# Attention, routed experts and gated layers on one core: routing rewritten, expert blocks of 224 tokens

## The chip, the core and the metric

The kernel runs on one core of a Trainium2 chip. A core has five engines with instruction streams of their own: TensorE (PE in the rows; its weight loads are PEld), VectorE (DVE), ScalarE (ACT), GpSimd (POOL) and SyncE (SP, which here only issues DMAs). They meet through semaphores. The metric is the device time of one execution in microseconds, lower is better. Before the change it was 645.58 us, the median of 3 runs (645.01 to 647.66).

## The reference, cut to what matters

```python
# 1. linear attention with decay: r, k, v are [4, 8, 768, 48]; gives x [3072, 384]
# 2. one expert of eight for each token, and only where x @ w_skip > 0
skip_score = x @ w_skip
do_compute = skip_score > 0
xc = x[do_compute]
logits = xc @ w_gate                      # [n, 8]
e_idx = np.argmax(logits, axis=1)
probs = softmax(logits); gate_w = probs[arange, e_idx]
for e in range(8):
    mask = e_idx == e
    h = np.maximum(xc[mask] @ w1[e], 0.0)         # 384 -> 1024
    y[mask] = gate_w[mask, None] * (h @ w2[e])    # 1024 -> 384
out[do_compute] = xc + y
# 3. gated layers on all 3072 tokens
h = (x @ m_w1) * (x @ m_w2) @ w3          # 384 -> 1024 -> 1024
return h @ w_out                          # 1024 -> 384
```

On its own inputs the reference sends 1490 of the 3072 tokens to an expert; the eight experts get 190, 182, 205, 159, 189, 184, 188 and 193 of them.

## The kernel before, in words

Four stages follow each other, each a block of its own; at a block's end all engines wait for each other.

**Attention** works through tiles of 128 rows in a software pipeline (`schedule`). Each finished tile is stored to `xbuf` in DRAM by SP, and TensorE makes nine logits a token from it (eight experts and the skip score). The last part of `lg` is put together when the last tile's logits are there.

**The fold** is independent of the tokens: w3 @ w_out is formed once as `wf`, in 8 chunks of 128 rows. `Fold.turn` transposes chunk i on TensorE (8 transposes), `turned` copies it out on ScalarE, `product` multiplies it by w_out (8 matmuls in four quarters), `taken` copies the result out. Product i waits until product i-1 has been taken. Chunk 0 is turned and multiplied at the end of attention, chunks 1 to 5 are multiplied in routing (1 to 7 turned), chunk 6 after the experts, chunk 7 in the gated layers. The fold's work stands between the steps of routing on TensorE in an order written out by hand.

**Routing** gives each routed token a slot: expert e owns slots from 256e on, and tokens over 256 of an expert go to overflow blocks. VectorE finds the best expert of each token (`mine`, one 0/1 number for each expert and 128 tokens), TensorE counts (ranks within a column, totals), VectorE turns the counts into a slot number `dest` in a chain of small steps, each waiting for the one ahead (`chain`), and splits it into a high part (`hi`, which group of 128 slots) and a low part (`lo`). From them come one-hot tables `oh_hi` and `oh_lo`; `vals` is `oh_hi` times each of five numbers of a token (two make up its number, three its gate), two on VectorE and three on GpSimd (`slot_values`). 24 matmuls `oh_lo` x `vals` then give the lists `slot_token` and `slot_gate`. GpSimd gathers the first expert's tokens by `slot_token` (indirect DMA, two of 128 rows), TensorE transposes them (L1132) and the experts begin.

**Experts**: for each of 8 experts `hidden` (L1146) runs 72 matmuls of 256 columns in four groups of 18, `outputs` (L1159) 2 x 24 matmuls of 384 columns, with the next expert's 6 transposes between the two halves. All are float32r with the operands split in a high and a low part. ScalarE makes the high parts, VectorE the low parts (`hidden_lo`: w2_lo and h_lo for each group; then `w1_lo_`, `x_lo`, `new`), and GpSimd gathers and scatters (`exchange`) and splits one block of the next stage's weights an expert (`wm_lo_`, in experts 0 to 5).

**Gated layers** then run over all tokens in 6 blocks of 512.

## Time and profile before

| | us |
|---|---|
| median of 3 runs | 645.58 |
| the profiled execution's own time | 649.34 |
| its span, first to last instruction | 647.6 |
| attention, up to the block's end | 0 to 138.5 |
| routing, up to the first expert's transposes | 138.8 to 178.5 |
| experts, up to the end of the last outputs | 178.5 to 322.6 |
| the fold's product 6, scatters, gated layers | 322.6 to 647.6 |
| TensorE busy | 613.1 (95%) |

The profiled execution is 3.76 us longer than the median of the runs, and 1.76 us of it lie outside the span. TensorE's granted clock was 1.00 (2.4 GHz) nearly everywhere and 0.50 (1.2 GHz) from 119.5 to 133.1 us. A plain f32 matmul shows as two rows in the timeline (the 8 matmuls of a product are x16), a transpose or a float32r matmul as one.

### The profile page before, as it was taken

The page shows a single profiled execution, that of the slowest core. Times are in us where ns is not written, and L with a number is a line of the kernel's source. Part 1 is how long each engine was busy: PE and PEld are TensorE (multiplying, and loading weights), DVE is VectorE, ACT ScalarE, POOL GpSimd, SP SyncE. Part 2 cuts the span into 40 slices and gives each one's busy share as a digit, 9 for nine tenths or more (in the row PEclk, how much of TensorE's full clock was granted, in tenths as well). Part 3 has the DMA queues.
Part 4 walks back from the last instruction along what each step waited for, and adds up shares of the span by engine and source line. Part 5 has one row for each costly group of instructions (what it writes and reads, how often), then busy time and mean ns, then how long its engine had stood idle before and what let it go on. Part 6 is the DMA issues. An engine that isn't in the chain of part 4 may idle for free. (4 is left out here: it accounts for less than half of the span.)

```text
span 647.6 us, 17433 instructions
## 1 busy us (share of the span) xinstructions
PE 613.1 (95%) x7362; PEld 548.0 (85%) x7362; DVE 302.6 (47%) x464; ACT 217.2 (34%) x382; POOL 155.6 (24%) x182
## 2 busy tenths in 40 slices
PE   7698998689999999999989999999999999999997
PEld 6688888645699999999958898888889888888886
DVE  5477878239377777778412232223214123223222
ACT  2144444212455555555232132122213123213212
POOL 6566777125514444333122000000000000000000
PEclk9899999689999999999999999999999999999999
DMA  9679999546156677764040003002002001001001
GB/s 133 115 145 188 190 187 211 157 128 254 51 172 221 249 266 259 251 222 164 19 153 1 0 1 99 0 1 98 1 1 97 1 1 49 1 0 50 1 0 50
DMA packets 104058, 67.77 MB, mean 105 GB/s; under 512 B 79459, under 2 KB 98053, under 8 KB 104017
## 3 DMA queue, kind: packets, MB, share of 16 engines
q1 hardware_dynamic: 75824, 57.88, 30.8%
q10 hardware_dynamic: 26144, 4.74, 4.3%
q0 software_dynamic: 2048, 4.58, 1.9%
q8 instruction: 29, 0.48, 0.3%
q14 instruction: 13, 0.10, 0.1%
HBM read 56.31 MB, written 12.58 MB: 106 GB/s over the span
## 5 line engine op out<-in xcount | busy, mean ns | idle before, releaser
L1443 DVE TENSOR_TENSOR gl_g_sb<-gl_a_sb,gl_pab 128x512 f32<-128x512 f32 x48 | 33.0, 688 | 187.0 <-ACT gl_a_sb L1420 187.0
L1363 PE MATMUL gl_pab<-gl_xT_hi,wm_lo 128*128 128x512 f32 x288 | 112.9, 392 | 0.0
L1363 PE MATMUL gl_pab<-gl_xT_lo,wm_hi 128*128 128x512 f32 x288 | 112.8, 392 | 0.0
L1363 PE MATMUL gl_pab<-gl_xT_hi,wm_hi 128*128 128x512 f32 x288 | 112.3, 390 | 0.0
L1420 ACT ACTIVATE gl_a_sb<-gl_pab 128x512 f32<-128x512 f32 x48 | 28.7, 597 | 185.2 <-PE gl_pab L1363 185.2
L1378 PE MATMUL gl_po<-gl_wf_hi,gl_g_hi 128*128 128x384 f32 x192 | 65.6, 342 | 0.7 <-DVE gl_g_lo L1445 0.7
L1378 PE MATMUL gl_po<-gl_wf_hi,gl_g_lo 128*128 128x384 f32 x192 | 64.7, 337 | 0.0
L1378 PE MATMUL gl_po<-gl_wf_lo,gl_g_hi 128*128 128x384 f32 x192 | 64.5, 336 | 0.0
L1363 PEld LDWEIGHTS gl_pab<-gl_xT_hi,wm_lo 128*128 128x128 f32 x288 | 54.0, 188 | 11.4
L1363 PEld LDWEIGHTS gl_pab<-gl_xT_lo,wm_hi 128*128 128x128 f32 x288 | 54.0, 188 | 10.6
L1363 PEld LDWEIGHTS gl_pab<-gl_xT_hi,wm_hi 128*128 128x128 f32 x288 | 54.1, 188 | 10.4
L1146 PE MATMUL ex_ph<-ex_xT_hi,ew_w_hi 128*128 128x256 f32 x192 | 54.3, 283 | 0.0
L1146 PE MATMUL ex_ph<-ex_xT_lo,ew_w_hi 128*128 128x256 f32 x192 | 54.2, 283 | 0.0
L1146 PE MATMUL ex_ph<-ex_xT_hi,ew_w_lo 128*128 128x256 f32 x192 | 53.9, 281 | 0.0
L1228 DVE TENSOR_TENSOR ew_w_lo<-ew_w_in,ew_w_hi 128x768 fp32r<-128x768 f32 x32 | 45.6, 1424 | 11.7 <-ACT ew_w_hi L1194 11.3
L1445 DVE TENSOR_TENSOR gl_g_lo<-gl_g_sb,gl_g_hi 128x512 fp32r<-128x512 f32 x48 | 33.8, 705 | 33.5 <-ACT gl_g_hi L1423 33.5
L1159 PE MATMUL ex_py<-ew_w_hi,ex_h_hi 128*128 128x384 f32 x128 | 44.1, 345 | 0.3 <-DVE ex_h_lo L1231 0.3
L1159 PE MATMUL ex_py<-ew_w_hi,ex_h_lo 128*128 128x384 f32 x128 | 43.0, 336 | 0.0
L1159 PE MATMUL ex_py<-ew_w_lo,ex_h_hi 128*128 128x384 f32 x128 | 43.0, 336 | 0.0
L1423 ACT ACTIVATE gl_g_hi<-gl_g_sb 128x512 fp32r<-128x512 f32 x48 | 30.3, 632 | 36.2 <-DVE gl_g_sb L1443 36.2
L1378 PEld LDWEIGHTS gl_po<-gl_wf_hi,gl_g_hi 128*128 128x128 f32 x192 | 36.1, 188 | 2.5 <-DVE gl_g_lo L1445 1.0
L1378 PEld LDWEIGHTS gl_po<-gl_wf_lo,gl_g_hi 128*128 128x128 f32 x192 | 36.1, 188 | 1.4
(198 smaller groups left out, 1143.3 us busy)
## 6 DMA issues: line engine op xcount, KB each, us to landing
ew_w_in<-in_moe_w SPq DMA_DIRECT2D x16, 1536.0 KB
w_in<-in_moe_w SPq DMA_DIRECT2D x14, 512.0 KB, 4.7
k_in<-in_k SPq DMA_DIRECT2D x48, 96.0 KB
v_in<-in_v ACTq DMA_DIRECT2D x48, 96.0 KB
r_in<-in_r SPq DMA_DIRECT2D x48, 96.0 KB
xbuf<-x_nat SPq DMA_DIRECT2D x24, 192.0 KB
gl_x_in<-xbuf SPq DMA_DIRECT2D x12, 384.0 KB, 4.2
out<-gl_o_sb SPq DMA_DIRECT2D x12, 384.0 KB, 2.5
```

Source lines behind the costliest of these rows:

```text
L1146: m = pe.matmul(p_h[g][:, f % 2, :], a[:, k, cols], b[:, k, :], start=(k == 0 and n == 0), stop=(k == KD - 1 and n == 2))
L1159: m = pe.matmul(p_y[i][:, 0:DM], a[:, f, cols], b[:, f, :], start=(f == 0 and n == 0), stop=(f == KF - 1 and n == 2))
L1228: dve.tensor_tensor(flat(w2_lo[:, 2 * g:2 * g + 2, :]), flat(w2_in[:, 2 * g:2 * g + 2, :]), flat(w2_hi[:, 2 * g:2 * g + 2, :]), ALU.subtra ...
L1363: m = pe.matmul(p_ab[f % 2][w][:, :], a[:, w * KD + k, cols], b[t.slot][:, k, :], start=(k == 0 and n == 0), stop=(k == KD - 1 and n == 2))
L1378: m = pe.matmul(p_o[i][:, 0:DM], a[f % 2][:, cols], b[:, f, :], start=(f == 0 and n == 0), stop=(f == KF - 1 and n == 2))
L1420: act.activation(a_sb[f % 2][:, :], p_ab[f % 2][0][:, :], ACT.Copy).then_inc(s_a, 1)
L1423: act.activation(g_hi[f % 2][:, :], g_sb[f % 2][:, :], ACT.Copy).then_inc(s_ghi, 1)
L1443: dve.tensor_tensor(g_sb[f % 2][:, :], a_sb[f % 2][:, :], p_ab[f % 2][1][:, :], ALU.mult).then_inc(s_g, 1)
L1445: dve.tensor_tensor(g_lo[f % 2][:, :], g_sb[f % 2][:, :], g_hi[f % 2][:, :], ALU.subtract).then_inc(s_glo, 1)
```

## The change

The tables that routing needs (`Tables`; 9 iotas, 6 memsets and one affine_select) are filled by GpSimd at the end of attention. Routing's VectorE chain is shorter: a scan over `mine` runs ahead of TensorE's counts, which then give the rank in the expert and the slot in one go (seven small matmuls in place of two). The first lists hold only the token's number (two of the five values, one of them made by ScalarE), the gates follow in a second run of 24 matmuls later. GpSimd makes one `vals`, issues the gathers, and then makes the two others; the split of the first expert's w1 moves from GpSimd to VectorE. The fold's product 0 moves from attention to routing, and its transposed chunks have four buffers in place of two. An expert's own block is 224 slots wide (`ROOM`; its slots still begin at 256e), so all its matmuls, copies, gathers and scatters shrink from 256 to 224 tokens (rows 128 + 96); tokens over 224 of one expert go to overflow blocks of 256.

```diff
@@ attention, TensorE
                 if f is other_rows and at(c, j, NT):
                     fold.turn(pe, 0, [p_AU[:, i, :] for i in range(2)])
-                if f is x_transposes and at(c, j, NT + 2):
-                    fold.product(pe, 0, p_AU[:, 0, :], (0,))
-                if f is logits and at(c, j, NT + 3):
-                    fold.product(pe, 0, p_AU[:, 0, :], (1, 2, 3))
@@ attention, GpSimd
             schedule(pool, ((products, 2), (new_state, -1), (values, 0)), 2, 0)
+            env["tables"].fill(pool)
@@ routing, SyncE
-                fold.load(sp, [2, 3])
+                fold.load(sp, [2])
                 ex.load_w1(sp, 0)
-                fold.load(sp, [4])
+                fold.load(sp, [3])
                 ex.load_w2(sp, 0)
-                fold.load(sp, [5, 6, 7])
+                fold.load(sp, [4, 5, 6, 7])
@@ routing, GpSimd
                 pool.wait_ge(s_slot, 1)
-                for i in range(DVE_VALS, 5):
-                    slot_values(pool, i)
-                ex.first_w1_lo(pool)
+                slot_values(pool, 2, piece[:, 0, :], s_gval)
                 pool.wait_ge(s_table, 1)
                 for i in range(2):
-                    ex.gather(pool, xbuf, 0, i, env["slot_token"][:, i:i + 1])
+                    ex.gather(pool, xbuf, 0, i, env["slot_token"][0:ex.rows(i), i:i + 1])
+                for i in range(1, 3):
+                    slot_values(pool, 2 + i, piece[:, i, :], s_gval)
@@ routing, TensorE
+                fold.product(pe, 0, p_W[0], (0, 1))
                 fold.turn(pe, 1, p_T[1])
-                fold.product(pe, 1, p_W[1], (0, 1))
-                pe.wait_ge(s_m, 1)
-                pe.matmul(p_rank, before[:, :], m16, start=True, stop=True)
-                pe.matmul(p_tot, ones[:, :], m16, start=True, stop=True).then_inc(s_mm, 1)
+                pe.wait_ge(s_m, 2)
+                for p in (p_pos, p_slot):
+                    pe.matmul(p, tb.before[:, :], mine, start=True, stop=False, skip_group_check=True)
+                    m = pe.matmul(p, tb.ones[:, :], earlier[:, :], start=False, stop=(p is p_pos), skip_group_check=True)
...
+                fold.product(pe, 0, p_W[0], (2, 3))
+                fold.product(pe, 1, p_W[1])
+                fold.turn(pe, 2, p_T[0])
+                pe.wait_ge(s_near, 1)
+                for h in range(2):
+                    pe.wait_ge(s_token, 2 + h)
+                    for t in range(h * NT // 2, (h + 1) * NT // 2):
+                        m = pe.matmul(p_list[:, 0:2 * NSL], oh_lo[:, t, :], vals[:, t, 0:2, :].rearrange("p v s -> p (v s)"),
+                                      start=(t == 0), stop=(t == NT - 1))
+                m.then_inc(s_list, 1)
@@ routing, ScalarE
+                act.wait_ge(s_slot, 1)
+                act.activation(vals[:, :, 1, :], oh_hi[:, :, :], ACT.Copy, scale=tb.row[:, 0:1]).then_inc(s_near, 1)
+                ex.first_w1_hi(act)
@@ routing, VectorE (the chain from the counts on)
+                tt(is_over[:, :, :], p_tot.unsqueeze(2).broadcast_to([P, E, NO]), tb.threshold[:, :].unsqueeze(1).broadcast_to([P, E, NO]), ALU.is_gt)
                 chain(dve.tensor_reduce(n_blocks[:, :], is_over[:, :, :], AX.X, ALU.add))
+                chain(dve.tensor_tensor_scan(ends[:, :], tb.one8[:, :], n_blocks[:, :], 0.0, ALU.mult, ALU.add))
                 tt(jump[:, :], ends[:, :], n_blocks[:, :], ALU.subtract)
+                chain(dve.scalar_tensor_tensor(jump[:, :], jump[:, :], float(CAP), tb.e_jump[:, :], ALU.mult, ALU.add))
+                chain(dve.scalar_tensor_tensor(over[:, :, :], eacht(p_pos), float(ROOM), over_t(jump[:, :]), ALU.is_ge, ALU.mult))
+                tt(pos[:, :, :], over[:, :, :], eacht(p_slot), ALU.add)
+                tt(pos[:, :, :], pos[:, :, :], eacht(mine), ALU.mult)
                 chain(dve.tensor_reduce(dest[:, :], by_t(pos[:, :, :]), AX.X, ALU.add))
@@ experts
+    ROOM = 7 * P // 4
+        def width(t):
+            return CAP if isinstance(t, Over) else ex.ROOM
-                                    m = pe.matmul(p_h[g][:, f % 2, :], a[:, k, cols], b[:, k, :],
+                                    m = pe.matmul(p_h[g][:, f % 2, 0:width(t)], a[:, k, cols], b[:, k, 0:width(t)],
```

How the instructions stand in a row shows the change of order. First TensorE, from the end of attention to the first run of list matmuls; before the change:

```order
L269 MATMUL p_K<-ident,x_nat 128x64 x6
L88 MATMUL p_AU<-wo,w3T 128x384 x2
L312 MATMUL p_Y<-w_gates,xT 64x9 x24
L88 MATMUL p_AU<-wo,w3T 128x384 x6
L116 UNCONDITIONAL_BRANCH
L756 UNCONDITIONAL_BRANCH
L68 MATMUL ro_pT<-ident,w_in 128x128 x8
L88 MATMUL ro_pW<-wo,w3T 128x384 x4
L763 MATMUL ro_p_count<-ro_mine,ro_before 128x192
L764 MATMUL ro_p_count<-ro_mine,ro_ones 128x192
```

TensorE at the same place after the change (`tb_` are the tables, `ro_pW` takes the fold's products, `ro_p_count` the counts):

```order
L269 MATMUL p_K<-ident,x_nat 128x64 x6
L312 MATMUL p_Y<-w_gates,xT 64x9 x24
L116 UNCONDITIONAL_BRANCH
L768 UNCONDITIONAL_BRANCH
L88 MATMUL ro_pW<-wo,w3T 128x384 x4
L68 MATMUL ro_pT<-ident,w_in 128x128 x8
L774 MATMUL ro_p_count<-tb_mine,tb_before 128x192
L775 MATMUL ro_p_count<-ro_earlier,tb_ones 128x192
L774 MATMUL ro_p_count<-tb_mine,tb_before 128x192
L775 MATMUL ro_p_count<-ro_earlier,tb_ones 128x192
L776 MATMUL ro_p_count<-tb_e_base,tb_ones 128x192
L778 MATMUL ro_p_count<-tb_mine,tb_ones 128x8
```

The 8 matmuls of product 0 left attention; half of them stand ahead of the counts, and half behind.

VectorE, from the slot numbers to the first copy out of the lists, before:

```order
L804 TENSOR_TENSOR ro_dest_i<-ro_dest,ro_g_r 128x24
L857 TENSOR_SCALAR ro_lo_i<-ro_dest_i 128x24
L858 CAST ro_lo<-ro_lo_i 128x24
L859 TENSOR_SCALAR ro_hi_i<-ro_dest_i 128x24
L860 CAST ro_hi<-ro_hi_i 128x24
L804 TENSOR_TENSOR ro_oh_hi<-ro_col,ro_hi 128x912
L864 TENSOR_TENSOR ro_oh_lo<-ro_col,ro_lo 128x3072
L694 TENSOR_TENSOR ro_vals<-ro_oh_hi,ro_val 128x24x38 x2
```

VectorE at the same place after the change:

```order
L876 SCALAR_TENSOR_TENSOR ro_dest_i<-ro_closed,ro_dest 128x24
L877 TENSOR_SCALAR ro_hi_i<-ro_dest_i 128x24
L878 CAST ro_hi<-ro_hi_i 128x24
L834 TENSOR_TENSOR ro_oh_hi<-tb_col,ro_hi 128x960
L729 TENSOR_TENSOR ro_vals<-ro_oh_hi,tb_first 128x24x40
L883 TENSOR_SCALAR ro_lo_i<-ro_dest_i 128x24
L884 CAST ro_lo<-ro_lo_i 128x24
L887 TENSOR_TENSOR ro_oh_lo<-tb_col,ro_lo 128x1536 x2
```

The low part moved behind `oh_hi` and the one `vals` that VectorE still makes, and `oh_lo` comes in two halves.

GpSimd, from the last piece of the gate to the first expert's gathers, before:

```order
L743 CAST ro_val<-ro_rest 128x24
L694 TENSOR_TENSOR ro_vals<-ro_oh_hi,ro_val 128x24x38 x3
L949 TENSOR_TENSOR ew_w_lo<-ew_w_in,ew_w_hi 128x3x256 x2
L954 DMA ew_x_in<-xbuf,slot_token 128x384 x2
L965 COPY ew_gate<-slot_gate 128x2
```

GpSimd at the same place after the change:

```order
L757 CAST ro_piece<-ro_rest 128x24
L729 TENSOR_TENSOR ro_vals<-ro_oh_hi,ro_piece 128x24x40
L983 DMA ew_x_in<-xbuf,slot_token 128x384
L983 DMA ew_x_in<-xbuf,slot_token 96x384
L729 TENSOR_TENSOR ro_vals<-ro_oh_hi,ro_piece 128x24x40 x2
L994 COPY ew_gate<-slot_gate 128x2
```

The gathers moved ahead of two of the three `vals`, the second one takes 96 rows, and the two splits of w1 are gone from this engine.

## Rows read from the trace of the kernel before

**Rows 1.** The page, part 1: TensorE's busy time, share of the span, instructions.

```profile
PE 613.1 (95%) x7362; PEld 548.0 (85%) x7362; DVE 302.6 (47%) x464; ACT 217.2 (34%) x382; POOL 155.6 (24%) x182
```

**Rows 2.** Windows: stretch, length; busy us (count) by engine; granted clock, DMA share, GB/s.

```profile
126.30:129.80 3.50, 3.50 (x50) 3.03 (x50) 0.56 (x1) 1.91 (x4) 0.00 (x0) 0.50 0.27 58
...
178.50:322.60 144.10, 143.78 (x1023) 142.21 (x1024) 106.97 (x125) 76.03 (x114) 47.72 (x42) 1.00 0.57 205
322.60:647.60 325.00, 317.90 (x1545) 276.31 (x1544) 85.00 (x127) 78.62 (x136) 8.78 (x9) 1.00 0.09 30
```

**Rows 3.** Timeline of TensorE, routing: start, length, operation [idle before, releaser].

```profile
130.15 2.93 PE L88 MATMUL p_AU<-wo,w3T 128*128 128x384 f32 x4
...
155.62 1.04 PE L68 MATMUL ro_pT<-ident,w_in 128*128 128x128 f32 x8
156.49 5.36 PE L88 MATMUL ro_pW<-wo,w3T 128*128 128x384 f32 x16
161.69 1.04 PE L68 MATMUL ro_pT<-ident,w_in 128*128 128x128 f32 x8
...
167.76 2.16 PE L772 MATMUL ro_p_list<-ro_vals,ro_oh_lo 128*128 128x190 bf16 x24
...
178.50 0.88 PE L1132 MATMUL ex_px<-ident,ew_x_in 128*128 128x128 f32 x6 [1.66 <-DMA ew_x_in<-xbuf,slot_token]
```

**Rows 4.** Waits of SyncE, 100 to 220 us: total, times, longest.

```profile
SPq L264 <- DMA xbuf<-x_nat: 2.1, 1, 2.1
```

**Rows 5.** Timeline of SyncE's issues and of ScalarE at the end of attention.

```profile
123.69 7.10 SPq L255 DMA_DIRECT2D xbuf<-x_nat  x4
...
138.04 0.49 ACT L96 ACTIVATE wf<-p_AU 128x384 f32<-128x384 f32 x1 [3.80 <-PE p_AU L88]
```

**Rows 6.** Timeline of VectorE, routing.

```profile
145.76 0.36 DVE L835 COPY ro_tot<-ro_p_count 128x192 f32<-128x192 f32 x1 [0.15 <-DVE ro_gate L830]
...
148.71 0.17 DVE L804 TENSOR_TENSOR ro_jump<-ro_jump,ro_e_base 128x8 f32<-128x8 f32 x1
...
154.25 3.36 DVE L864 TENSOR_TENSOR ro_oh_lo<-ro_col,ro_lo 128x3072 bf16<-128x3072 bf16 x1
157.53 5.15 DVE L694 TENSOR_TENSOR ro_vals<-ro_oh_hi,ro_val 128x912 bf16<-128x912 bf16 x2
...
162.77 1.58 DVE L804 TENSOR_TENSOR ro_done<-ro_ends,ro_over_block 128x88 f32<-128x88 f32 x1
```

**Rows 7.** Timeline of GpSimd, routing.

```profile
154.31 9.94 POOL L694 TENSOR_TENSOR ro_vals<-ro_oh_hi,ro_val 128x912 bf16<-128x912 bf16 x3 [7.03 <-DVEq L863]
```

**Rows 8.** Timeline of TensorE, experts 2, 3, 6 and 7 (first matmul of each step).

```profile
216.23 0.28 PE L1146 MATMUL ex_ph<-ex_xT_hi,ew_w_hi 128*128 128x256 f32 x1
...
224.87 0.34 PE L1159 MATMUL ex_py<-ew_w_hi,ex_h_hi 128*128 128x384 f32 x1
...
229.04 0.82 PE L1132 MATMUL ex_px<-ident,ew_x_in 128*128 128x128 f32 x6
...
233.87 0.28 PE L1146 MATMUL ex_ph<-ex_xT_hi,ew_w_hi 128*128 128x256 f32 x1
...
287.45 0.28 PE L1146 MATMUL ex_ph<-ex_xT_hi,ew_w_hi 128*128 128x256 f32 x1
...
305.62 0.28 PE L1146 MATMUL ex_ph<-ex_xT_hi,ew_w_hi 128*128 128x256 f32 x1
```

**Rows 9.** Timeline of TensorE's weight loads after a wait, gated layers.

```profile
641.52 0.19 PEld L1378 LDWEIGHTS gl_po<-gl_wf_hi,gl_g_hi 128*128 128x128 f32 x1 [1.01 <-DVE gl_g_lo L1445]
641.63 0.19 PEld L1378 LDWEIGHTS gl_po<-gl_wf_lo,gl_g_hi 128*128 128x128 f32 x1
```

**Rows 10.** Timeline of VectorE and GpSimd in expert 3.

```profile
236.65 0.96 DVE L1228 TENSOR_TENSOR ew_w_lo<-ew_w_in,ew_w_hi 128x768 fp32r<-128x768 f32 x1 [1.97 <-ACT ew_w_hi L1194]
...
238.13 3.73 DVE L1228 TENSOR_TENSOR ew_w_lo<-ew_w_in,ew_w_hi 128x768 fp32r<-128x768 f32 x1
...
238.65 2.39 POOL L1100 TENSOR_TENSOR wm_lo<-w_in,wm_hi 128x1024 fp32r<-128x1024 f32 x1
```

More of the change, by code:

```diff
@@ L622, in routing @@
     lg = env["lg"]
+    tb = env["tables"]
     with ExitStack() as ctx:
@@ L766, in _ @@
-                for i in range(2, 6):
-                    fold.turn(pe, i, p_T[i % 2])
-                    if i > 2:
-                        fold.product(pe, i - 1, p_W[(i - 1) % 2])
-                pe.wait_ge(s_oh, 6)
+                pe.wait_ge(s_m, 2)
+                for p in (p_pos, p_slot):
+                    pe.matmul(p, tb.before[:, :], mine, start=True, stop=False, skip_group_check=True)
+                    m = pe.matmul(p, tb.ones[:, :], earlier[:, :], start=False, stop=(p is p_pos), skip_group_check=True)
@@ new lines, in _ @@
+                pe.matmul(p_slot, tb.ones[0:1, :], tb.e_base[0:1, :, :].rearrange("p e t -> p (e t)"), start=False, stop=True, skip_group_check=True)
+                last = [x.rearrange("p (e t) -> p e t", t=NT)[:, :, NT - 1] for x in (mine, earlier[:, :])]
+                pe.matmul(p_tot, tb.ones[:, :], last[0], start=True, stop=False, skip_group_check=True)
+                pe.matmul(p_tot, tb.ones[:, :], last[1], start=False, stop=True, skip_group_check=True).then_inc(s_mm, 1)
+                fold.product(pe, 0, p_W[0], (2, 3))
@@ L771, in _ @@
+                fold.turn(pe, 3, p_T[1])
+                fold.product(pe, 2, p_W[0])
+                fold.turn(pe, 4, p_T[0])
+                fold.product(pe, 3, p_W[1])
+                pe.wait_ge(s_table, 1)
+                pe.wait_ge(s_gval, 3)
                 for t in range(NT):
-                    m = pe.matmul(p_list[:, 0:5 * NSL], oh_lo[:, t, :], vals[:, t, :, :].rearrange("p v s -> p (v s)"),
+                    m = pe.matmul(p_list[:, 2 * NSL:5 * NSL], oh_lo[:, t, :], vals[:, t, 2:5, :].rearrange("p v s -> p (v s)"),
@@ L782, in _ @@
                 act.wait_ge(s_exp, 1)
                 act.activation(expo[:, :, :].rearrange("p e t -> p (e t)"), dif[:, :, :].rearrange("p e t -> p (e t)"), ACT.Exp).then_inc(s_exp, 1)
+                fold.turned(act, 1, p_T[1])
+                fold.taken(act, 0, p_W[0])
+                act.wait_ge(s_slot, 1)
+                act.activation(vals[:, :, 1, :], oh_hi[:, :, :], ACT.Copy, scale=tb.row[:, 0:1]).then_inc(s_near, 1)
+                ex.first_w1_hi(act)
                 fold.taken(act, 1, p_W[1])
-                for i in range(2, 6):
+                fold.turned(act, 2, p_T[0])
@@ L867, in _ @@
-                for i in range(DVE_VALS):
-                    slot_values(dve, i)
+                for h in range(2):
+                    ts = slice(h * NT // 2, (h + 1) * NT // 2)
+                    dve.tensor_tensor(oh_lo[:, ts, :], tb.col[:, :].unsqueeze(1).broadcast_to([P, NT // 2, P]),
+                                      lo[:, ts].unsqueeze(2).broadcast_to([P, NT // 2, P]), ALU.is_equal).then_inc(s_token, 1)
+                dve.wait_ge(s_list, 1)
+                chain(dve.tensor_copy(lst[:, 0, :], p_list[:, NSL:2 * NSL]))
@@ L916, with rows @@
 class ExpertInputs:
+    ROOM = 7 * P // 4
+    def rows(self, i):
+        return min(P, self.ROOM - i * P)
     def __init__(self, sb, sem, w1, w2):
@@ L1091, in exchange @@
                         if t.num() >= 0:
-                            ex.scatter(pool, xbuf, x_new[t.slot][:, i, :], tokens(t, i), s_out[t.slot])
+                            ex.scatter(pool, xbuf, x_new[t.slot][0:ex.rows(i), i, :], tokens(t, i), s_out[t.slot])
                     if nxt.inside(E):
@@ L1465, in program @@
     CAP = 2 * P
-    NO = (N - 1) // CAP
+    ROOM = ExpertInputs.ROOM
+    NO = max(j + (N - j * (ROOM + 1)) // CAP for j in range(1, E + 1))
     NSL = (E + NO) * CAP // P
```

255 lines of the change are left out of this document (128 added, 127 removed).

## The prediction

> **What bounds the kernel.** I read the page first: TensorE is busy 613.1 of 647.6 us [rows 1]. Then windows by stage: it is busy 143.78 of 144.10 us in the experts and 317.90 of 325.00 behind them [rows 2]. So time is to be had where TensorE does less or waits less, and another engine counts only where TensorE waits for it. The change leaves the last 325 us alone. It acts on three places: the end of attention, routing, and the 8 experts. For routing I read TensorE's timeline and asked at each gap who ends it; for the experts the start of each step, to get a cadence, and VectorE beside GpSimd.
>
> **End of attention.** Its block ends when ScalarE has taken product 0, at 138.04 + 0.49 = 138.5 us [rows 5]. Without the product the next to end is SyncE: its last stores are issued at 123.69 + 7.10 = 130.8, and it waits 2.1 us for them [rows 4, 5], so 132.9. The last logits need only one more tile's 12 small matmuls behind the stretch at 130.15 and are sooner done. Filling the tables lies under that, since GpSimd had nothing to do there. Routing began 0.3 us behind the block's end, so it now begins at 133.2 in place of 138.8: 5.6 us earlier. This is no gain by itself, because the product comes back on the same engine.
>
> **Routing, TensorE's work.** A turn takes 156.49 - 155.62 = 0.87 us, a product 161.69 - 156.49 = 5.20 [rows 3]. Now 6 products (31.2) and 7 turns (6.1). The lists took 2.16 us for 24 matmuls of 190 columns [rows 3]; two runs of 80 and 120 columns I put at 2.6 together, the seven counts at 0.5. Sum 40.4, so from 133.3 to 173.7 at full clock and with no wait.
>
> **Waits on that path.** The counts wait for VectorE's `mine` and scan, seven steps from 133.2 on (by the step costs below 3.3 us): ready at 136.5, and TensorE gets there at 133.3 + 2.6 + 0.87 = 136.8. No wait; that half of product 0 stands ahead of them is what hides it. Call this point C. From the counts' end to the slots VectorE's chain took 154.25 - 145.76 = 8.5 us [rows 6]. A step on 192 numbers costs 0.36 us plus 0.03, one on 8 numbers 0.17 [rows 6]; taken out are five of the first kind, one scan (0.6), two cheaper ones and two small ones, and the two steps for `lo` move behind: 3.6 in all, 4.9 stay. `oh_hi` is ready at C + 0.7 + 4.9 = C + 5.6.
>
> Next come one `vals` and two halves of `oh_lo`. VectorE and GpSimd exclude each other here: `done`, 88 numbers, took 1.58 us and ended at 164.35, GpSimd's three `vals` at 164.25 [rows 6, 7]; two `vals` on VectorE took 5.15, three on GpSimd 9.94, of which the first waited out `oh_lo` (3.36). I read that as 1.0 us of own time on VectorE and 1.6 on GpSimd, in turns. So: VectorE's `vals` 1.0, GpSimd's 1.6, then `oh_lo` 1.6 and 1.6. The second half is there at C + 11.4. TensorE comes with product 0's rest, 0.5 for product 1 waiting until 0 is taken, product 1, turn 2: at C + 9.6. It ends the lists at C + 12.1, where without either wait it would be C + 10.3: 1.8 us. The second run of lists needs GpSimd's other `vals`, done some 8 us behind the first gather, and TensorE has 12 us of fold ahead of it: covered; were that cover gone, each us late would cost one. The gathers leave at about C + 15, 24 us ahead of their use, where before they landed last and TensorE waited 1.66 us for them [rows 3]. The w1 split on VectorE (4 x 0.96) stands behind the token list and ahead of nothing urgent. Cost zero.
>
> **The clock.** TensorE's granted clock was 0.50 from 119.5 to 133.1 us, though TensorE was busy 3.50 of 3.50 us from 126.3 on with attention's small matmuls and transposes [rows 2]. It rose some 3 us after product 0's matmuls had begun at 130.15 [rows 3]. Now those begin at 133.3. I expect the rise 3 to 6 us later, take 4.4, and lose half: 2.2 us. Bounds: 0 (the rise comes under attention) and 9 (the rival below). The Trainium skill, "TensorE: Matmul & The Clock Gate", part 4 on PE-mode transpose, says that transposes do not count as busy for the clock; that window at 0.50, full of transposes and small matmuls, agrees. By that rule turn 1 would not bring the rise nearer, only the products around it would.
>
> Sum: 173.7 + 1.8 + 2.2 = 177.7. Behind it the last copy (0.5), the block's end (0.3) and the start (0.1): transposes at 178.6 against 178.50 [rows 3]. **Routing: +0.1 us**, between -2.1 (clock early) and +7. The product moved in costs what ending attention early gives.
>
> **Experts, columns.** Hidden's 72 matmuls take 224.87 - 216.23 = 8.64 us [rows 8], 0.120 each: 256 columns at 2.4 GHz are 0.107, and 0.013 more. If only the columns counted, 224 would give 0.107. But each matmul has weights of its own, and a load is not free: after a wait the first load starts at 641.52 and the next, which begins when the first matmul runs, at 641.63 [rows 9]. So a load takes about 0.11 us, more than 224 columns (0.093). Bounds for the cadence: 0.107 (columns) and 0.120 (a load of 0.107 with the same 0.013 on top). I take 0.110, the row's own load time: 72 x 0.010 = 0.72 us an expert. The half of the transposes with 96 columns gives 0.08 (3 x 0.03). Outputs stream 384 columns of w2 as before, with fewer weights: nothing.
> By the Trainium skill, "TensorE: Matmul & The Clock Gate", section on LDWEIGHTS, a load takes its columns / 1.2 ns, 107 ns for 128, whatever the rows. The trace's 0.11 agrees; taken with a fixed 13 ns it would leave hidden at 0.120 and the saving at nothing, which is my third case.
>
> **Experts, VectorE.** TensorE's period was 233.87 - 216.23 = 17.64 us, but 305.62 - 287.45 = 18.17 late in the stage [rows 8]: it waits there for h_lo. The cause is seen in expert 3: w2_lo takes 3.73 us where the one ahead took 0.96, until GpSimd's wm_lo ends at 241.04 [rows 10]. VectorE's round (w2_lo and h_lo behind that, w1_lo, x_lo, x_new, which starts GpSimd's next exchange) lasts about 18.1 us. Shorter h_lo, x_lo (64 columns, 0.07 each) take 0.3 off it. So experts 2 to 6 can't run at TensorE's 17.64 - 0.80 = 16.84. Sum: lead 2.35, two at 16.84, one at 17.5, four at 17.8, the last 16.26: 141.0 against 144.1 [rows 2]: **-3.1 us**. Without that cover 6.4 + 1.2 (the waits before) = 7.6.
>
> **Overflow.** The largest expert has 205 tokens, under 224: no extra block.
>
> **Total** -3.0 us. The profiled execution took 649.34, 1.76 outside its span and 3.76 over the median; it would be 646.3, the span 644.6. Runs without these 3.76 us: 645.58 - 3.0 = **642.6 us**.
>
> **Rivals.**
> *Full saving (638.0).* VectorE falls out of step with GpSimd, so that no w2_lo meets wm_lo: -7.6. For it: the one collision shown takes 2.8 us, and a shift of less could avoid it. Against: the period grows over the stage, so what is late stays late.
> *Weights bound hidden (644.7).* Cadence stays 0.120; only transposes (0.6) and shorter VectorE steps (0.4) remain, less 0.1. For it: load and stream are equal at 256 columns. Against: the isolated load shows no fixed part on top.
> *Slower: the clock stays low (about 650).* Routing's products are now cut by the counts and by the wait for the lists. If TensorE stays at 1.2 GHz until the lists, 152 in place of 137.7, it loses (152 - 137.7) / 2 = 7.2 us, giving 649.8. It decides from a rise at about 149.5 on.
> *Slower: a float32r matmul under 256 columns runs like plain f32 (about 793).* No row has one. A plain product takes 5.36 us for 16 passes of 384 columns [rows 3], 0.85 ns a column and pass, two passes: 0.38 us for 224; 576 x 0.26 = 150 us on top. It breaks everything at the first hidden.
>
> **Chances.** Forecast 0.45 (own range 641 to 644.5), full saving 0.20, weights 0.25, clock 0.06, plain f32 0.04. The range 637.5 to 647.0 leaves out the two slow cases and the tails. Half a per cent, 3.2 us, is what a measurement of this kernel tells from no change: faster means under 642.4, which is full saving and half the forecast, 0.42; same is the other half and the weights' case, 0.48; slower 0.10.
>
> **What would show it.** Attention's block ending near 133 with SyncE last; clock 1.00 from 136 to 140; the first lists ending about 12 us behind the counts; transposes at 178.6 with no wait for the gather; hidden in 7.9 us; periods of 16.8 that grow to 17.8, with w2_lo at 3 us and more. Hidden at 8.6, no growing period, or TensorE waiting over 3 us in routing would make it wrong.

## The result: slower, 654.1 us in place of 646.3

The changed kernel took 654.14 us, the median of 4 runs (653.16 to 655.33), against 646.29 for the kernel before in the same session (645.01 to 647.66): ratio 1.0122, 95% interval 1.0093 to 1.0151. A second session gave 653.35, ratio 1.0121 (1.0096 to 1.0145). I had forecast 642.6 and a range up to 647.0, so the time lies outside it, on the side to which I gave 0.10.

First TensorE's windows by stage, after the change; the columns are those of [rows 2].

```profile
133.00:179.17 46.17, 43.25 (x208) 27.77 (x208) 23.73 (x41) 14.82 (x26) 12.02 (x14) 0.95 0.42 143
179.17:323.61 144.44, 142.38 (x1022) 134.41 (x1023) 101.89 (x123) 72.66 (x114) 47.33 (x42) 1.00 0.57 204
333.90:652.50 318.60, 313.66 (x1520) 272.09 (x1520) 84.35 (x126) 78.18 (x135) 7.82 (x8) 1.00 0.09 28
```

The last stretch, the gated layers from their first transposes on, is not a window of [rows 2]; this is its window in the kernel before.

```profile
332.88:647.60 314.72, 309.76 (x1520) 271.99 (x1520) 84.39 (x126) 78.13 (x135) 7.80 (x8) 1.00 0.09 29
```

Up to the transposes the two traces differ by 0.67 us (179.17 against 178.50), in the experts by 0.34 (144.44 against 144.10), and by 3.88 in the gated layers, whose code, instruction counts and data are the same. The first question is therefore not routing at all. TensorE's timeline there, first the changed kernel and then the one before: the first of 18 matmuls of 512 columns, and the first of the 384-column ones behind them.

```profile
400.89 0.40 PE L1408 MATMUL gl_pab<-gl_xT_hi,wm_hi 128*128 128x512 f32 x1
...
405.09 0.34 PE L1423 MATMUL gl_po<-gl_wf_hi,gl_g_hi 128*128 128x384 f32 x1
```

```profile
405.20 0.39 PE L1363 MATMUL gl_pab<-gl_xT_hi,wm_hi 128*128 128x512 f32 x1
...
409.32 0.33 PE L1378 MATMUL gl_po<-gl_wf_hi,gl_g_hi 128*128 128x384 f32 x1
```

18 matmuls take 4.20 us in place of 4.12. From start to start, over all 864 of them, it is 233.3 ns in place of 228.7: 864 x 4.6 ns = 4.0 us. TensorE waits no longer there (318.60 - 313.66 = 4.9 us, and 314.72 - 309.76 = 5.0 before); the matmuls themselves are slower, at full clock.

Routing in the changed kernel, TensorE's timeline (answers to [rows 3]):

```profile
130.42 0.53 PE L312 MATMUL p_Y<-w_gates,xT 64*64 64x9 f32 x24 [0.21 <-ACT xT L457]
132.98 5.19 PE L88 MATMUL ro_pW<-wo,w3T 128*128 128x384 f32 x8 [2.03 <-PEq L116]
138.01 1.04 PE L68 MATMUL ro_pT<-ident,w_in 128*128 128x128 f32 x8
138.89 0.25 PE L774 MATMUL ro_p_count<-tb_mine,tb_before 128*128 128x192 bf16 x1
...
139.56 2.83 PE L88 MATMUL ro_pW<-wo,w3T 128*128 128x384 f32 x8
143.06 5.40 PE L88 MATMUL ro_pW<-wo,w3T 128*128 128x384 f32 x16 [0.67 <-ACT wf L96]
...
149.70 0.59 PE L787 MATMUL ro_p_list<-ro_vals,ro_oh_lo 128*128 128x80 bf16 x12 [0.37 <-DVE ro_oh_lo L887]
151.28 0.60 PE L787 MATMUL ro_p_list<-ro_vals,ro_oh_lo 128*128 128x80 bf16 x12 [0.99 <-DVE ro_oh_lo L887]
...
179.17 0.78 PE L1169 MATMUL ex_px<-ident,ew_x_in 128*128 128x128 f32 x6 [0.90 <-PEq L730]
```

Product 0's first half took 138.01 - 132.98 = 5.03 us where the second, at full clock, took 2.6. The granted clock was 0.50 over it, 1.2 GHz; the window is 131.0 to 137.8:

```profile
131.00:137.80 6.80, 4.82 (x8) 2.73 (x9) 4.71 (x11) 0.59 (x2) 1.70 (x4) 0.50 0.70 240
```

In the experts the hidden step now takes 8.0 us in place of 8.64, as forecast, but the periods (hidden's first matmul to the next expert's) are 17.05, 17.03, 18.38, 18.81, 18.77, 17.99, 17.89, where they had been 17.6 to 18.2 [rows 8]. Three of them are the loss. Expert 3, the counterpart of [rows 10]: SyncE's issues of the loads, ScalarE, VectorE, GpSimd, and the DMA queues from 227.2 to 236.7.

```profile
227.26 0.38 SPq L969 DMA_DIRECT2D ew_w_in<-in_moe_w  x1
227.91 0.36 SPq L1106 DMA_DIRECT2D w_in<-in_moe_w  x1
...
236.67 1.06 ACT L1253 ACTIVATE wm_hi<-w_in 128x1024 f32 x1 [6.12 <-DMA w_in<-in_moe_w]
...
238.49 3.35 DVE L1268 TENSOR_TENSOR ew_w_lo<-ew_w_in,ew_w_hi 128x768 fp32r<-128x768 f32 x1 [3.89 <-ACT ew_w_hi L1233]
...
238.60 2.42 POOL L1136 TENSOR_TENSOR wm_lo<-w_in,wm_hi 128x1024 fp32r<-128x1024 f32 x1
```

```profile
q1 hardware_dynamic: 1392, 2.95, 89.7%
q8 instruction: 1, 0.02, 0.7%
```

ScalarE takes wm_hi and then w2_hi, in this order. wm_hi waits for the last piece of the two loads, 236.67 - 227.26 = 9.41 us behind the first issue; in the kernel before that was 7.9 to 8.3 in all six experts. Here already the first w2_lo meets wm_lo and is held to 3.35 us, where in [rows 10] one had gone ahead in 0.96. The q8 row is what differs: one fetch of code, a single packet of 16 KB that took 1.13 us, at 232.3, in the middle of the load. What the delay costs is seen at TensorE's weight loads for `outputs` of this expert: three groups in a row wait for VectorE's h_lo.

```profile
243.83 0.19 PEld L1197 LDWEIGHTS ex_py<-ew_w_hi,ex_h_hi 128*128 128x128 f32 x1 [0.39 <-DVE ex_h_lo L1272]
...
245.23 0.19 PEld L1197 LDWEIGHTS ex_py<-ew_w_hi,ex_h_hi 128*128 128x128 f32 x1 [0.41 <-DVE ex_h_lo L1272]
...
246.63 0.19 PEld L1197 LDWEIGHTS ex_py<-ew_w_hi,ex_h_hi 128*128 128x128 f32 x1 [0.41 <-DVE ex_h_lo L1272]
```

### The profile page after: what moved, and what is told of

Its sections match the earlier page's. It is cut to its first block and busy times, and to the rows that moved or that the text cites. A ratio compares the mean times of both kernels' runs of the same rounds, so it can differ in the third digit from the quotient of the medians.

```text
span 652.5 us, 17487 instructions
## 1 busy us (share of the span) xinstructions
PE 618.4 (95%) x7391; PEld 543.1 (83%) x7391; DVE 295.1 (45%) x456; ACT 215.1 (33%) x383; POOL 149.1 (23%) x183
## 5 line engine op out<-in xcount | busy, mean ns | idle before, releaser
L1408 PE MATMUL gl_pab<-gl_xT_hi,wm_lo 128*128 128x512 f32 x288 | 114.8, 398 | 0.0
L1408 PEld LDWEIGHTS gl_pab<-gl_xT_lo,wm_hi 128*128 128x128 f32 x288 | 54.1, 188 | 12.1
L1268 DVE TENSOR_TENSOR ew_w_lo<-ew_w_in,ew_w_hi 128x768 fp32r<-128x768 f32 x32 | 45.6, 1426 | 19.3 <-ACT ew_w_hi L1233 18.6
L1183 PE MATMUL ex_ph<-ex_xT_hi,ew_w_hi 128*128 128x224 f32 x192 | 52.8, 275 | 0.0
L1183 PE MATMUL ex_ph<-ex_xT_lo,ew_w_hi 128*128 128x224 f32 x192 | 52.8, 275 | 0.0
L1183 PE MATMUL ex_ph<-ex_xT_hi,ew_w_lo 128*128 128x224 f32 x192 | 52.7, 275 | 0.0
L1197 PE MATMUL ex_py<-ew_w_hi,ex_h_hi 128*96 128x384 f32 (+1 forms) x128 | 45.5, 355 | 2.1 <-DVE ex_h_lo L1272 0.9
L1197 PE MATMUL ex_py<-ew_w_lo,ex_h_hi 128*96 128x384 f32 (+1 forms) x128 | 43.2, 338 | 0.0
L1197 PE MATMUL ex_py<-ew_w_hi,ex_h_lo 128*96 128x384 f32 (+1 forms) x128 | 43.2, 337 | 0.0
L983 POOL DMA_INDIRECT ew_x_in<-xbuf,slot_token x16 | 18.1, 1133 | 88.8 <-DVE ex_x_new L1295 66.0
```

What stands on the lines that cost most here:

```text
L983: pool.indirect_dma_start(self.x_in[slot][0:tokens.shape[0], i, :], None, xbuf[:, :], bass.IndirectOffsetOnAxis(ap=tokens, axis=0), bounds ...
L1183: m = pe.matmul(p_h[g][:, f % 2, 0:width(t)], a[:, k, cols], b[:, k, 0:width(t)], start=(k == 0 and n == 0), stop=(k == KD - 1 and n == 2))
L1197: m = pe.matmul(p_y[i][0:n_tok, 0:DM], a[:, f, cols], b[:, f, :], start=(f == 0 and n == 0), stop=(f == KF - 1 and n == 2))
L1268: dve.tensor_tensor(flat(w2_lo[:, 2 * g:2 * g + 2, :]), flat(w2_in[:, 2 * g:2 * g + 2, :]), flat(w2_hi[:, 2 * g:2 * g + 2, :]), ALU.subtra ...
L1408: m = pe.matmul(p_ab[f % 2][w][:, :], a[:, w * KD + k, cols], b[t.slot][:, k, :], start=(k == 0 and n == 0), stop=(k == KD - 1 and n == 2))
```

## Experiments

The kernels ran beside the kernel before (645.4 to 646.2 us in these sessions). A ratio difference of 0.001 is 0.65 us; each interval is about 0.002 to either side.

| run | median us | ratio to before [95%] |
|---|---|---|
| again (before, unchanged) | 645.39 | 0.9988 [0.9961, 1.0015] |
| after_again (after, unchanged) | 653.35 | 1.0121 [1.0096, 1.0145] |
| after_32 | 646.76 | 1.0022 [1.0003, 1.0040] |
| before_32 | 649.35 | 1.0049 [1.0031, 1.0067] |
| before_10880 | 646.54 | 1.0002 [0.9982, 1.0022] |
| gl_pad | 644.35 | 0.9967 [0.9944, 0.9990] |
| shift_176 | 661.71 | 1.0255 [1.0218, 1.0292] |
| w2_first | 644.56 | 0.9988 [0.9967, 1.0008] |
| wm_dve | 642.98 | 0.9967 [0.9944, 0.9990] |
| best | 639.95 | 0.9909 [0.9889, 0.9929] |
| best_256 | 645.89 | 0.9990 [0.9971, 1.0010] |
| before_best | 642.33 | 0.9954 [0.9937, 0.9970] |
| after_256 | 656.46 | 1.0175 [1.0148, 1.0202] |
| p0_att | 638.96 | 0.9904 [0.9882, 0.9926] |

### Addresses: 32 bytes

The tables are allocated ahead of all tensors of attention, experts and gated layers, and the fold's two further buffers shift everything by 8192 bytes. So attention's r, k, v and the gated xT, which had started at 128 bytes past a multiple of 256, now start at 224 past one. Nothing in the diff's logic says this; the addresses do.

```diff
         env["tables"] = Tables(*scope(c, "tb_"), N // P, E, NSL, CAP, ROOM, NO, S)
+        sb("pad", [P, 8])          # after_32: 32 bytes a partition; before_32: the same line in the kernel before
```

> The changed kernel with a dummy tensor of 32 bytes a partition behind the tables, so that the experts' weights and all tensors of the gated layers start on a multiple of 64 bytes again, as they did before the change (the tables left them 32 bytes off). Theory P (placement: a 512-column matmul streams more slowly from an xT that starts 32 bytes off): the gated 512-column matmuls go from 233 ns back to 229, 864 of them, -4.0 us; the stage takes 314.7 us in place of 318.6. The experts' xT goes from 0 to 32 bytes off, so hidden may lose some of its 0.1115 us a matmul: at most 576 x 0.007 = 4 us. Total 650 to 652. Rival Q (the 4 us come from wm_hi and wm_lo lying 8 KB higher, or from anything else than the 32 bytes): no change, 654.

> The kernel before with the same 32 bytes of dummy ahead of the experts' and the gated layers' tensors, so that the gated xT is 32 bytes off and the experts' xT is on a multiple of 64. Theory P: gated 512-column matmuls from 229 to 233 ns, +4.0 us; hidden's 256-column matmuls, which stream xT, go from 120 ns to nearer 110, so hidden takes up to 0.6 us less an expert, though the VectorE and GpSimd round may keep the period. Total 646 to 650. Rival Q: both stages as before, 646.

32 bytes of nothing took 6.4 us (by ratios, 1.0022 against 1.0121) to 7.4 (by medians) off the changed kernel and put 3 to 4 on the one before. In before_32 the gated matmuls went to 233.1 ns, as theory P said; rival Q is out. In two points P was wrong. Hidden did not care where the experts' xT starts: 8.52 us from first to last start with 256 columns in both kernels before, 7.92 with 224 in both after. And in after_32 the gated matmuls only went to 232.1 ns, 864 x 1.2 ns = 1.0 us. Of the rest of the gain a part is one that I had not looked for, in attention. These are the rows of queue q1 (packets, MB, share of 16 engines) over the first 120 us, of the kernel before, the changed one, after_32, before_32 and before_10880:

```profile
q1 hardware_dynamic: 55451, 16.17, 65.7%
```

```profile
q1 hardware_dynamic: 55355, 16.04, 76.4%
```

```profile
q1 hardware_dynamic: 55472, 16.20, 60.3%
```

```profile
q1 hardware_dynamic: 55472, 16.20, 70.7%
```

```profile
q1 hardware_dynamic: 55472, 16.20, 59.5%
```

The same packets and bytes take 60 to 76% of the engines' time. Most are packets of 192 bytes, and their mean time, from all records, follows the start of their tensors past a multiple of 256 bytes: 16.0 ns at 0 (after_32, before_10880), 17.5 at 128 (before, again), 19.3 at 160 (before_32), 20.6 to 21.8 at 224 (after, after_again, after_256). Routing began at 132.8, 133.4 and 131.5 us in the three traces of the changed routing at 224, and at 128.5 to 130.9 (mean 129.5) in the six at 0: about 3 us.

That the slower packets make these 3 us is likely, but not shown in the old code: there routing began at 138.8 and 137.7 us with the tensors at 128, at 136.1 with them at 160, and at 136.8 and 130.7 in two traces at 0. The last two (before_10880, before_best) have the same attention at the same addresses and differ by 6.0 us; in the one TensorE's granted clock was 0.50 for 20 us of it, in the other for 7. The clock has a part in the medians too. Each execution's mean granted clock is on record; twice its distance from 1, times the span, is the time at half clock: 26 us on the mean in the changed kernel, 20 in after_32, 16 in the kernel before. Among 136 executions, each compared with the others of its own run, a us more at half clock goes with 0.21 us more of time. By this estimate 1.3 of the 6.4 us came with the clock; whether slower packets lower it was not tested. Nor is the whole gain placed: in the traces the experts took 144.4 us in the changed kernel and 140.3 in after_32, with one period over 18.3 in place of three; the second trace of the changed kernel has two and gl_pad two as well, so nothing ties that to the addresses.
The Trainium skill, "DMA: Bandwidth & Descriptors", section on how a descriptor splits into AXI transactions, says that a transaction starts on a 256-byte boundary, so that a piece which crosses one needs a second. It says so of the reading side. On the writing side the trace agrees in one point: 0, where the pieces of r and v (two thirds of the packets, laid 256 bytes apart) cross no boundary, is the fastest. At 128, 160 and 224 all of them cross one, and yet these three differ, so the rule does not give the order, and no run here tells the mechanism.

> The kernel before with 10880 bytes of dummy, so that attention's tensors lie where after_32 has them (119296) and the gated layers' too, but wm_hi and wm_lo stay (59264). Theory P (addresses alone): attention's packets of 192 bytes take 16.1 ns on the mean in place of 17.7 and its block ends 2 to 4 us sooner; gated 512-column matmuls 232 ns in place of 228.7 (+2.9 us), since xT lies off by 2688 bytes within 4096. Total 644 to 647. Rival (the shorter attention of after_32 came from the change itself, its tables on GpSimd or product 0 gone from it): attention and its packets as in before; then total 649.

```diff
+        sb("pad", [P, 2720])       # 10880 bytes, ahead of attention's tensors in the kernel before
```

Packets at 16.0 ns and gated matmuls at 232.1, both as theory P had it, in the old code. So it is neither the tables nor the moved product. The loss behind (864 x 3.4 ns = 2.9 us) does not show in the median, 646.5, so about as much was gained elsewhere, to 1.3 us either way. before_32 gives no such sum: its 3 to 4 us are what its gated layers alone lose (3.8), though its packets are slower than those of the kernel before.

> after_32 with 1408 bytes of dummy ahead of the gated layers' tensors alone, so that they start at 120704, the same place within 4096 bytes as before the change (108416). In after_32 they start on a multiple of 64 but the 512-column matmuls still take 232.1 ns on the mean and not before's 228.7. Theory P2 (it is not only the 32 bytes: where xT lies within some KB against the weights wm_hi and wm_lo sets the rest): back to 228.7, 864 times, -2.9 us. Rival (wm_hi and wm_lo lie 8 KB higher than before, and that is what costs): 232 stays, no change. Rival 2 (another offset, above 4096 bytes, matters): something else between 227 and 233.

```diff
+        sb("pad_gl", [P, 352])     # 1408 bytes, behind the experts' scope
         gated_layers(nc, env, xbuf, out)
```

TensorE in gl_pad, the same pair of matmuls as above:

```profile
394.18 0.39 PE L1408 MATMUL gl_pab<-gl_xT_hi,wm_hi 128*128 128x512 f32 x1
...
398.30 0.33 PE L1423 MATMUL gl_po<-gl_wf_hi,gl_g_hi 128*128 128x384 f32 x1
```

4.12 us again, 228.7 ns on the mean; even the sequence of single intervals (230, 233, 236, 224, 231, ...) is that of the kernel before. P2 holds and the 8 KB under wm_hi don't matter. What counts is where the gated layers' tensors, xT among them, start: 1920 bytes into a stretch of 4096 gives 228.7 ns (before and gl_pad), 512 gives 232.1, 1952 gives 233.1, 480 gives 233.3. That the stretch is 4096 bytes is not shown: gl_pad and the kernel before lie 12288 apart, which 256 divides as well, and past a multiple of 256 the four places are 128, 0, 160 and 224. Nor is it shown which tensor it is, since all move together; xT is what the slower matmuls stream. Why was not found. The total of gl_pad fell by 2.4 us (medians) to 3.6 (ratios) against after_32, for 2.9 expected.

### Experts: a fetch of code in the load

> after_32 with 176 more instructions on TensorE that do nothing (352 waits on a semaphore that is already there, packed two by two) at the end of attention, where TensorE waits for SyncE anyway. They only move TensorE's later code. In after_32 two 16 KB fetches of code begin at 226.7 and 243.9, in the middle of the loads of w2 and the next stage's weights, and those two loads take 9.1 and 8.9 us in place of 7.6 to 8.0. Theory F (the fetch holds up one of the 16 DMA engines for 1 us, the last piece of the load lands late, ScalarE's wm_hi and w2_hi and with them VectorE's w2_lo fall behind GpSimd's wm_lo): the fetches move 10 us ahead or 4.5 us behind, all loads take 8.1 or less, and the period of 18.7 us goes: experts 1.0 to 1.7 us shorter. Rival (VectorE's round is simply longer than TensorE's; the late landing is a companion): periods as in after_32 (17.03 four times, 18.7, 17.8, 17.8). The waits themselves may cost routing up to 2 us, so the experts' stage is read, not the total.

```diff
+            for _ in range(352):
+                pe.wait_ge(env["s_iota"], 2)     # end of attention, TensorE
```

The issue of the load, ScalarE's wm_hi and VectorE's first two w2_lo in expert 3, and TensorE's first step of routing:

```profile
236.95 0.38 SPq L971 DMA_DIRECT2D ew_w_in<-in_moe_w  x1
...
244.81 1.06 ACT L1255 ACTIVATE wm_hi<-w_in 128x1024 f32 x1 [4.36 <-DMA w_in<-in_moe_w]
...
246.64 0.96 DVE L1270 TENSOR_TENSOR ew_w_lo<-ew_w_in,ew_w_hi 128x768 fp32r<-128x768 f32 x1 [2.13 <-ACT ew_w_hi L1235]
248.05 3.75 DVE L1270 TENSOR_TENSOR ew_w_lo<-ew_w_in,ew_w_hi 128x768 fp32r<-128x768 f32 x1
```

```profile
144.86 4.55 PE L88 MATMUL ro_pW<-wo,w3T 128*128 128x384 f32 x8 [19.44 <-PEq L116]
```

The fetches moved to 213.0, 230.8 and 248.5, between the loads, and all six loads landed in 7.7 to 8.2 us. In the ten traces in which nothing but the load releases wm_hi there are 60 loads: the 12 in which a fetch began 2.4 to 4.4 us ahead of wm_hi took 8.9 to 9.7 us from issue to wm_hi, the other 48 took 7.6 to 8.3. So the fetch delays the load: shown. And with the load in time (7.86 us here) the first w2_lo goes ahead again and the second is held, as in [rows 10]. But the periods became 17.05, 17.03, 17.03, 17.46, 17.6, 18.03, 17.66, their sum 121.9 in place of 122.4: of the 1.0 to 1.7 us that I expected, 0.5 came. VectorE's round still holds the experts at 17.5 to 18.0, only the 18.7 is gone. The Trainium skill, "Runtime: NRT & Kernel Launch", section on instruction fetch, says that code comes in blocks of 16 KiB and the cost of a crossing is mostly hidden. The block is what the trace shows; for the rest, TensorE, whose code it is, waits in these experts only for VectorE's h_lo, and it is ScalarE that waits for the delayed load.
The time to do nothing was mis-sized: SyncE had issued its last store at 124.6, so nearly all of TensorE's 19.44 us are the 176 instructions, 0.11 us each, and the total is no result.

> after_32 with one step of ScalarE moved: the first w2_hi of an expert no longer stands behind wm_hi, which waits for the later of the two loads. Theory F: the late landing no longer reaches VectorE; the first w2_lo runs 1.5 us sooner and never falls behind wm_lo: periods at most 17.8, experts 1.0 to 2.5 us shorter than after_32's 140.3. Rival (VectorE's round limits): no change in the periods.

```diff
-  rounds(act, whole(act, (hidden_hi, 0), (w1_hi_, 1), (x_hi, 1), (wm_hi_, 0)), ...)
+  rounds(act, whole(act, (lambda t: w2_part(t, 0), 0), (wm_hi_, -1), (hidden_hi, 0), (w1_hi_, 1), (x_hi, 1)), ...)
```

Periods 17.03, 17.03, 17.03, 17.75, 17.84, 16.97, 17.03; the experts take 138.6 us in place of 140.3, 1.7 less. The rival is out: VectorE's round is not the limit as such. (The edit also takes the load's wm_hi one place later, behind the first w2_hi.) What holds it is seen in VectorE's rows: the first w2_lo is early, the second is held by wm_lo.

```profile
230.74 0.96 DVE L1269 TENSOR_TENSOR ew_w_lo<-ew_w_in,ew_w_hi 128x768 fp32r<-128x768 f32 x1 [1.11 <-ACT ew_w_hi L1234]
...
233.38 3.82 DVE L1269 TENSOR_TENSOR ew_w_lo<-ew_w_in,ew_w_hi 128x768 fp32r<-128x768 f32 x1
```

> after_32 with wm_lo (the low part of a block of the gated layers' weights) moved from GpSimd, where it costs 2.4 us and holds VectorE's w2_lo for 2.8, to VectorE, one expert later, behind the two x_new, where VectorE waits for ScalarE for 2 us and more. Theory (the collision of w2_lo and wm_lo is all that keeps the experts from TensorE's own 17.03 us): all seven periods 17.03, experts' stage 137.1 us in place of 140.3, total 3.2 us under after_32. Rival (VectorE has too much to do with 1.3 us more of its own): periods of 17.5 and more, no gain.

```diff
-  (GpSimd, behind exchange)  wm_lo_(Item(t // 2, t % 2, 0, 2))
+  rounds(dve, whole(dve, (hidden_lo, 0), (w1_lo_, 1), (x_lo, 1), (new, 0), (wm_lo_, -1)), 2, E, 1, 0)
```

```profile
245.53 0.61 DVE L1289 SCALAR_TENSOR_TENSOR ex_x_new<-ex_py,ew_gate,ew_x_in 96x384 f32<-96x384 f32 x1 [2.21 <-PE ex_py L1191]
246.07 1.21 DVE L1295 TENSOR_TENSOR wm_lo<-w_in,wm_hi 128x1024 f32 x1
247.71 0.96 DVE L1262 TENSOR_TENSOR ew_w_lo<-ew_w_in,ew_w_hi 128x768 fp32r<-128x768 f32 x1 [0.43 <-ACT ew_w_hi L1227]
```

All periods are 17.03 to 17.05, TensorE's own, and the total fell by 3.6 us (ratios) to 3.8 (medians) against after_32, for 3.2 expected, though two of its six loads still took 9.1 us. wm_lo costs VectorE 1.21 us in a gap, where on GpSimd it had held w2_lo for 2.8. The stage, whole, is TensorE at work without a gap, in 137.75 us (the window begins with the transposes):

```profile
175.04:312.79 137.75, 137.75 (x1023) 134.77 (x1024) 97.41 (x129) 74.19 (x114) 40.02 (x36) 1.00 0.59 214
```

With wm_lo off GpSimd no period grew in any of the five traces (wm_dve, best, best_256, before_best, p0_att: 17.03 to 17.05 with 224 tokens, 17.63 to 17.72 with 256): the collision is what lets it grow. It need not: in before_10880, with wm_lo on GpSimd, all periods were 17.63 to 17.72 too.

### The parts of the change on equal ground

> The changed kernel with all three: 32 bytes of dummy behind the tables, 1408 bytes ahead of the gated layers' tensors, wm_lo on VectorE one expert later. Expected from the parts: wm_dve's 643.0 less gl_pad's 2.9 (864 matmuls from 232.1 to 228.7 ns) = 640.0; periods 17.03 seven times; under both kernels. Rival (the parts overlap): 642 or more.

> The kernel best with expert blocks of 256 tokens. What do blocks of 224 bring where nothing but TensorE sets the experts' pace? Theory: periods of 17.63 in place of 17.03, first and last step alike: 8 x 0.6 = 4.8 us, total 4.8 over best. Rival (the 224 blocks bring nothing even then): no difference.

> The kernel before with the three edits of best: tensors at best's addresses (10880 and 1408 bytes of dummy), wm_lo on VectorE. Against best_256 it tells what the rewritten routing is worth, and against best what the whole change is worth on equal ground. Theory (routing +0.1 as I predicted, blocks of 224 -4.8): before_best 644.7, equal to best_256 and 4.7 over best. Rival (the rewritten routing costs 3 us and more, which placement doesn't explain): before_best 642 or less.

```diff
-    ROOM = 7 * P // 4
+    ROOM = 2 * P               # best_256
```

best is both paddings and wm_dve in one, 639.95 us for 640.0 expected, 0.9% under the kernel before. best against best_256 is the blocks of 224 alone: -0.0081, 5.2 us (4.8 expected). best_256 against before_best is the rewritten routing: +0.0036, 2.3 us by ratios and 3.6 by medians, with intervals that put it between 0.6 and 4.0. I had expected 0.1, so before_best came out near the rival's number. Where these 2.3 us are lost stays open.
The whole change with both paddings and wm_lo off GpSimd is best against before_best: -0.0045, -2.9 us (-4.6 to -1.2). That it equals my forecast of -3.0 is luck: the forecast was made for kernels in which wm_lo holds w2_lo, and its parts were -3.1 and +0.1, not -5.2 and +2.3. The pair that keeps the collision, with attention's and the gated layers' tensors at the same addresses, is after_32 against before_10880: +0.0020, +1.3 us (-0.5 to +3.1). So with equal addresses too the change, as it was made, shows no gain.

> The changed kernel with expert blocks of 256 tokens (ROOM = 256), all the rest of the change kept, tensors at the changed kernel's addresses. Theory (the 224-token blocks bring TensorE 0.6 us an expert, which the later waits for h_lo take back): experts in 144 to 145 us, gated layers 318.6, total 654 (within 1 us of the changed kernel). Rival (the smaller blocks did save, and something else of the change costs 3 us in the experts): 657 or more.

This one came out at 1.0175 against the changed kernel's 1.0121, 3.5 us more (1 to 6): near the rival's number, though not for its reason. The theory that the smaller blocks' gain was wholly taken back is wrong; with 256 the fetches meet the loads as well (9.7 and 9.3 us, periods 18.7 and 19.25). Blocks of 224 gained some 3 us even at the bad addresses.

> The kernel best with the fold's product 0 back at the end of attention, its pieces where the kernel before has them, and routing's later products and turns set one place earlier so that TensorE has work ahead of the lists; all else of the new routing stays. In best the routing block took 47.1 us to the first transposes and TensorE's clock was at half for product 0's first half (5.0 us in place of 2.6), behind 2.3 us in which TensorE waited at the block's end. Theory R (product 0 costs more in routing than it saves in attention: it stands first behind the wait, at half clock): routing block 39 to 40 us, attention 4 to 6 us longer, total 1.5 to 3 us under best. Rival (what the product costs is the same at either place, as I predicted, and the 3.6 us between best_256 and before_best are lost elsewhere): the total of best, 640.

```diff
 (attention, TensorE)  + fold.product(pe, 0, p_AU[:, 0, :], (0,)) ... + fold.product(pe, 0, p_AU[:, 0, :], (1, 2, 3))
 (routing, TensorE)    - fold.product(pe, 0, p_W[0], (0, 1))       ... - fold.product(pe, 0, p_W[0], (2, 3))
```

TensorE in p0_att and in best, product 0 and the first expert's transposes:

```profile
128.73 4.14 PE L88 MATMUL p_AU<-wo,w3T 128*128 128x384 f32 x12
...
174.77 0.78 PE L1170 MATMUL ex_px<-ident,ew_x_in 128*128 128x128 f32 x6 [0.90 <-PEq L735]
```

```profile
130.30 5.46 PE L88 MATMUL ro_pW<-wo,w3T 128*128 128x384 f32 x8 [2.34 <-PEq L116]
...
176.82 0.78 PE L1163 MATMUL ex_px<-ident,ew_x_in 128*128 128x128 f32 x6 [0.90 <-PEq L730]
```

From the block's start (VectorE's first step, 133.70 and 130.15) routing takes 41.1 us in place of 46.7, and attention ends 3.6 later: 2.05 us sooner at the transposes. The direction is theory R's, the sizes are smaller than it said at both places. The medians differ by 1.0 and the ratios by 0.0005 with intervals of 0.002, so the gain is not shown beyond these two traces, and whether product 0's place has a part in the 2.3 us that the rewritten routing costs stays open.

> The kernel before, unchanged, to get a second trace of it. Its first profiled execution took 649.34 us, 3.0 us over its median. Theory 1 (that one execution was slow by chance, all its stages as usual): about 646, the gated layers from the transposes on again 314.7 us. Theory 2 (the profile itself costs time and the gated layers are shorter without it): again about 649 with a profile.

> The changed kernel once more, for a second trace and a ratio on this chip. Theory P (the loss is tied to its addresses): again 654, attention's packets of 192 bytes at 20 ns and more, gated 512-column matmuls at 233.3 ns, periods of 18.4 and more only in the experts whose loads hold a 16 KB fetch of code. Rival (chance of one execution): 646 to 650.

The two repeats: the kernel before took 648.5 profiled, gated layers 314.4 us, matmuls at 228.7 ns; so the total of theory 2 and the stages of theory 1. Theory 2 has the other runs against it: the 13 further profiled executions of the table lie between 2.6 us under and 2.1 over the median of their own run, 0.4 under on the mean. What made both of the kernel before's long stays open. The changed kernel had packets at 20.6 ns, 233.3 ns in the gated layers, and periods of 18.49 and 18.75 in just the two experts whose loads hold a fetch (9.3 and 9.5 us), at a total of 651.66. Theory P holds.

## Why the prediction was wrong, by its own steps

In terms of the profiled execution the forecast was a span of 644.6 and it was 652.5: 7.9 us. In terms of ratios I forecast -3.0 us and +7.8 came, 10.8 off: 6.4 of it left with the 32 bytes, 4.3 is still there between kernels with equal addresses (+1.3 for -3.0).

- **"The change leaves the last 325 us alone": failed, 3.9 us.** True of the instructions, false of the addresses: 864 matmuls at 233.3 ns in place of 228.7. I read the allocations of new tensors as free. gl_pad and before_32 show it from both sides.
- **Experts, VectorE: mis-sized, 144.4 in place of 141.0, 3.4 us.** Mechanism right (wm_lo holds w2_lo, TensorE waits, period above TensorE's). But I took the round as 17.8 from a trace in which one w2_lo always got ahead; when a fetch of code holds the load by 1.2 us, none does, and the round is 18.4 to 18.8, three times: 55.96 in place of 17.5 + 17.8 + 17.8 = 53.1, 2.9 us. The first two periods (17.05 and 17.03 in place of 16.84) add 0.4, the last two 0.3. My rival "full saving" by a lucky phase was the right question with the wrong sign.
- **Experts, columns: nearly right.** 224 columns gave 0.1115 us a matmul (0.110 taken), hidden 8.0 for 7.9; TensorE's own period fell by 0.60 in place of 0.80. The rivals "weights" and "plain f32" are out.
- **Routing: right by its parts in this trace, wrong in what it is worth.** Routing began at 132.8 (133.2 taken) with SyncE's stores last, product 0 at 132.98 (133.3), the clock's loss was 5.03 - 2.6 = 2.4 (2.2), waits 0.67 + 0.37 + 0.99 = 2.0 (1.8), first lists 12.1 us behind the counts, second lists and gathers without a wait, transposes at 179.17 (178.6). The rival "clock stays low" is out: it was back at 137.8. But the agreement at 132.8 is luck: I set a block end taken from a trace with faster packets against one with slower ones, and with the tensors at 0 routing began at 129.5 on the mean. Between kernels at the same addresses the rewritten routing costs 2.3 us (0.6 to 4.0) where I had +0.1: within my bounds, but with the cause open.
- **From the trace to the median: failed, 3.6 us.** I took 3.76 us off because the profiled execution of before was that much over its median, as if every profiled execution were. The changed kernel's was not (654.34 and 654.14). So the two traces differ by 4.9 us where the medians differ by 7.9. Attention's slower packets, about 3 us, would fill that gap, covered up by a long trace of before; this is argued, not shown.

Two readings were off without moving the forecast: 5.36 us for 16 passes of 384 columns is 0.87 ns a column and pass, not 0.85, and from C + 15 to 178.6 the gathers had some 27 us, not 24.

The slower cases had 0.10 between them, and none was this. I had listed mechanisms that act through time and engines only, and the one with the largest share acts through where things lie.
